# Products of ones at TensorE's waits in a threshold search, and twenty side products moved later

## The chip, the cores and the metric

The kernel runs on one core of one Trainium2 chip. The metric is the device time of one execution in microseconds. One core has five engines with queues of their own (TensorE, VectorE, ScalarE, GpSimd, SyncE) that meet at semaphores, and 16 DMA engines that are fed from queues of SyncE, ScalarE and GpSimd.

## The reference, cut to what is computed

```python
x = mlstm(q, k, v, i_gate, f_gate, o_gate)       # 3072 tokens x 320

# first mixture of experts: balanced, 8 experts, 384 tokens each
logits = x @ w_gate                               # 3072 x 8
order = np.argsort(-logits.flatten())
for idx in order:                                 # the greatest logit first
    tok, e = idx // E, idx % E
    if assigned[tok] >= 0 or counts[e] >= cap:
        continue
    assigned[tok] = e; counts[e] += 1
out[assigned == e] = relu(x[assigned == e] @ w1[e]) @ w2[e]

# second mixture of experts: x / |x| against expert_emb / |expert_emb|,
# argmax picks the expert, softmax gives its weight
out[idx == e] = gate_w * (relu(x[idx == e] @ w1[e]) @ w2[e])
```

## The kernel before, in words

It has four stages: the recurrence (mLSTM), the routing of the first mixture with its logits, the experts of the first mixture, the experts of the second. The change is in the routing alone.

The greedy assignment is done without a sort. It runs in 7 phases (`PHASES`). In a phase every token that is still free chooses its best open expert (VectorE, `keys`), and for each expert the smallest key that it can accept is searched 4 bits at a time in 8 rounds (`ROUNDS`). The 24 blocks of 128 tokens stand as 24 columns. One round is a ring between two engines:

- VectorE compares the keys with 16 candidates in three pieces, L1040, of 6, 10 and 8 blocks (`FIRST`, `cmp_ready`).
- TensorE counts: a product with the capacity, L1509, then 24 small products of 8 columns, L1513, each over one block of the comparison. The last one raises `cnt_ready`.
- VectorE tests the counts, L1074 (`kcol_ready`).
- TensorE turns the digits found into the next candidates: `digit`, L1497. Digits of earlier rounds of the same half (`q < r`) are added before the wait for `kcol_ready`, the new one behind it (`kb_ready`). In the first round of a half there is no earlier one, in its fourth there are three.
- VectorE compares against the result, which it reads from PSUM. In rounds 0 and 4 the candidates are a constant in SBUF instead.

After 8 rounds `settle` takes the tokens above the threshold and the ties in order. TensorE's part of it is `assign(0)` (L1475), a count (L1525), three products that rank the ties (L1528 to L1530) and one that sums them (L1531), then `assign(1)`.

Between these TensorE has side work, `side(count)`: 192 steps (L1489, two products of 8 columns each, which the trace shows as four records) that multiply the transposed `w2` of the first experts by the normalised embeddings of the second router. `made` counts them. Their operands come in 16 chunks of 12 steps, in four buffers. The last product of a chunk raises `w2t_used`, and SyncE loads chunk j into a buffer once `w2t_used` says that chunk j - 4 is done. After the last step ScalarE copies the sum (`w2e_ready`), which TensorE wants before it turns the rows of expert 0.

SyncE's queue is in order. Around the routing it holds: chunks 4, 5 and 6, the store of all tokens (`x_rows<-tokens`, L440), chunks 7 to 15, then the raw weights of expert 2 (L407 to L412). After the routing GpSimd gathers the rows of expert 0 (L731) by the order found, TensorE turns them (L1566) and the expert stage begins.

GpSimd splits the weights of experts 0 and 1 (L758 to L789) in two bursts during the routing.

`spin(dst, count)` (L1307 to L1310) issues products of a matrix of ones with 512 columns into a bank that nobody reads. Before the change it is used in the first 25 us alone. `bank[5]`, `bank[6]` and `bank[1]` are idle at the places where the change writes ones.

Of the kernel before, what the change touches and what calls it, by code (L numbers as in the profile page):

```python
# [87 lines left out]
def build(nc, t, out):  # L88
    ctx = ExitStack()
    with ctx:  # L90
# [196 lines left out]
        bank = [ctx.enter_context(nc.psum_tensor(f"bank{i}", [128, 512], fp32)) for i in range(8)]  # L287
# [1014 lines left out]
        def _(pe):  # L1302
# [4 lines left out]
            def spin(dst, count):  # L1307

                for _ in range(count):
                    T.matmul(dst[:, :], ones[:, :], ones[:, 0:1].to_broadcast([128, 512]), start=True, stop=True)  # L1310
# [158 lines left out]
            def ranks(src):  # L1469

                T.matmul(bank[4][:, 0:E * G], tri[:, :], src.rearrange("p e g -> p (e g)"), start=True, stop=False)
                return T.matmul(bank[4][:, 0:E * G], ones[:, :], prev_b.rearrange("p e g -> p (e g)"), start=False, stop=True)

            def assign(j, src, last=False):
                T.matmul(bank[0][:, 0:G * E], eye[:, j, :], src.rearrange("p g e -> p (g e)"), start=False, stop=last).then_inc(assigned_ready, 1)  # L1475
# [3 lines left out]
            def side(count):  # L1479

                if made[0] == 0:
                    pe.wait_ge(embT_done, 1)
                for m in range(made[0], made[0] + count):
                    f, k, j = m // KT, m % KT, m // (KT * FT // 2)
                    at = k * HF + f % (FT // 2) * 128
                    if m % (KT * FT // 2) == 0:
                        pe.wait_ge(ld_w2t[j % 4], 16 * (j // 4 + 1))
                    for rows in (slice(0, 64), slice(64, 128)):
                        last = T.matmul(bank[3][rows, f * E:(f + 1) * E], w2t[j % 4][:, at + rows.start:at + rows.stop], eg[:, k * E:(k + 1) * E],  # L1489
                                        start=(k == 0), stop=(k == KT - 1))  # L1490
                    if (m + 1) % (KT * FT // 2) == 0:
                        last.then_inc(w2t_used[j % 4], 1)
                made[0] += count

            def digit(q, last, r=None):
                r = q if last else r
                return T.matmul(threshold[r % 2][:, 0:WAYS], kcol[:, q:q + 1].to_broadcast([WAYS, 128]), kstep[:, last * ROUNDS + q, :],  # L1497
                                start=(q % (ROUNDS // 2) == 0), stop=bool(last))

            side(40)  # L1500
            pe.wait_ge(choice_ready, 1)
            T.matmul(bank[0][:, 0:G * E], eye[:, 0, :], over_b.rearrange("p g e -> p (g e)"), start=True, stop=False).then_inc(assigned_ready, 1)
            for ph in range(PHASES):
                for r in range(ROUNDS):
                    n = ph * ROUNDS + r
                    if r == 0:
                        pe.wait_ge(cap_ready, ph + 1)
                        pe.wait_ge(choice_ready, ph + 1)
                    T.matmul(bank[6][0:WAYS, 0:E], minus1[0:1, :], cap_eff[0:1, :], start=True, stop=False)  # L1509
                    for g in range(G):  # L1510
                        if g in FIRST:
                            pe.wait_ge(cmp_ready, PIECES * n + FIRST.index(g) + 1)
                        last = T.matmul(bank[6][0:WAYS, 0:E], cmp_b[:, g, :], choice[:, g, :], start=False, stop=(g == G - 1))  # L1513
                    last.then_inc(cnt_ready, 1)
                    for q in range(r // (ROUNDS // 2) * (ROUNDS // 2), r):
                        digit(q, 0, r)
                    pe.wait_ge(kcol_ready, n + 1)
                    digit(r, 1).then_inc(kb_ready, 1)
                    if r in (2, 5):
                        side(1)  # L1520
                side(3)
                pe.wait_ge(over_ready, ph + 1)
                assign(0, over_b)
                pe.wait_ge(osum_ready, ph + 1)
                T.matmul(bank[1][:, 0:E], ones[:, :], osum_b[:, :], start=True, stop=True).then_inc(over_count, 1)  # L1525
                side(2)
                pe.wait_ge(ties_ready, ph + 1)
                T.matmul(bank[4][:, 0:E * G], eye[:, 2, :], tie_b.rearrange("p e g -> p (e g)"), start=True, stop=False)  # L1528
                T.matmul(bank[4][:, 0:E * G], tri[:, :], tie_b.rearrange("p e g -> p (e g)"), start=False, stop=False)
                T.matmul(bank[4][:, 0:E * G], ones[:, :], prev_b.rearrange("p e g -> p (e g)"), start=False, stop=True)  # L1530
                T.matmul(bank[5][:, 0:E], ones[:, :], run_b[:, G - 1:E * G:G], start=True, stop=True).then_inc(rank_ready, 1)  # L1531
                side(3)
                pe.wait_ge(missed_ready, ph + 1)
                assign(1, missed_b)
                if ph < PHASES - 1:
                    side(7)
            pe.wait_ge(over_ready, PHASES + 1)
            assign(0, over_b, True)
            pe.wait_ge(ties_ready, PHASES + 1)
            ranks(chosen[:, :, :]).then_inc(rank_ready, 1)  # L1540
            side(20)
            for g in range(G):
                if g % (G // PIECES) == 0:
                    pe.wait_ge(lane_ready, g // (G // PIECES) + 1)
                last = T.matmul(bank[6][:, 0:2 * G], lane_is[:, g, :], place_of[:, g, :, :].rearrange("p a j -> p (a j)"), start=(g == 0), stop=(g == G - 1))
            last.then_inc(order_ready, 1)
# [215 lines left out]
```

## Time and profile before

| | before |
|---|---|
| times of 3 runs | 833.1, 836.4, 884.54 us; median 836.4 |
| the profiled execution | 834.51 us, its span 832.5 us |
| TensorE busy in the span | 732.9 us, 88% |
| mean granted TensorE clock | 0.875 |
| logits end, routing begins | 160.4 us |
| routing ends, rows of expert 0 turned | 320.2 us |

The profile is one execution. Its span runs from the first to the last instruction. Engines are called PE (TensorE), PEld (its weight loads), DVE (VectorE), ACT (ScalarE), POOL (GpSimd), SP (SyncE). A number in brackets behind a row is the time that the engine stood idle before it and what ended that. The granted clock is the share of 2.4 GHz that TensorE was given: 1.00 is 2.4 GHz, 0.50 is 1.2 GHz.

### The profile page before, as it was taken

What the parts mean: (1) busy time and instruction counts of PE and PEld (TensorE: products, weight loads), DVE (VectorE), ACT (ScalarE), POOL (GpSimd) and SP (SyncE); (2) the same over time, 40 slices, a digit from 0 to 9 for tenths busy, and PEclk for the clock granted to TensorE, in tenths of its full rate; (3) what the DMA queues carried; (4) which work ended last, traced back from release to release, by engine and by line L of the source; (5) the groups of instructions that cost most, each with busy time, mean ns of one, the idle gap of its engine ahead of it and who ended that gap; (6) DMA issues with size and microseconds to landing.
All of it is one profiled execution on the core that took longest, in us unless ns stands there. A gap on an engine that the chain in (4) does not pass through costs nothing.

```text
span 832.5 us, 21421 instructions
## 1 busy us (share of the span) xinstructions
PE 732.9 (88%) x7336; PEld 645.3 (78%) x7338; DVE 448.5 (54%) x1220; ACT 276.9 (33%) x625; POOL 419.0 (50%) x573
## 2 busy tenths in 40 slices
PE   7988889987888878999999999089999999999994
PEld 3677768975766757999999998068988988988994
DVE  7799997657666672366556665713222222222231
ACT  3444321000000002567666676323333332333330
POOL 4677772537000003578787766502644775347530
PEclk9999999855555556999999999689999999999997
DMA  5666685799321162335545533364749667642310
GB/s 170 205 220 206 224 272 155 187 311 331 101 80 67 41 178 58 99 99 191 168 128 186 188 122 107 113 176 122 231 131 299 189 209 224 189 133 80 111 56 0
DMA packets 66155, 132.28 MB, mean 159 GB/s; under 512 B 14743, under 2 KB 48432, under 8 KB 64306
## 3 DMA queue, kind: packets, MB, share of 16 engines
q1 hardware_dynamic: 45346, 84.85, 32.5%
q0 software_dynamic: 9600, 35.85, 13.9%
q10 hardware_dynamic: 11152, 10.82, 4.7%
q8 instruction: 36, 0.59, 0.3%
q14 instruction: 21, 0.17, 0.1%
HBM read 94.23 MB, written 15.34 MB: 132 GB/s over the span
## 4 chain that ended last, share of the span: by engine, by line
PE 60%; DVE 20%; issue 9%; ACT 3%; POOL 3%; DMA 2%; DVEq 1%; SPq 0%; ACTq 0%; POOLq 0%
PE bank L1552 10%; PE bank L1553 9%; PE bank L1554 9%; PE bank L1513 5%; PE bank L1579 3%; PE bank L1580 3%; PE bank L1581 3%; PE bank L1670 3%; DVE mlstm_arena L879 2%; PE bank L1445 2%; PE bank L1652 2%; PE bank L1651 2%; DVE routing_arena L1040 2%; PE bank L1489 2%; PE bank L1584 1%
## 5 line engine op out<-in xcount | busy, mean ns | idle before, releaser
L1552 PE MATMUL bank<-w_hi,hT_hi 128*128 (+1 forms) x440 | 141.2, 321 | 5.9 <-DVE hT_lo L1154 3.4
L1553 PE MATMUL bank<-w_lo,hT_hi 128*128 (+1 forms) x440 | 137.4, 312 | 0.0
L1554 PE MATMUL bank<-w_hi,hT_lo 128*128 (+1 forms) x440 | 137.1, 312 | 0.0
L789 POOL TENSOR_TENSOR w_lo<-w_raw,w_hi 128x320 fp32r<-128x320 f32 x128 | 109.0, 882 | 17.8 <-ACT w_hi L525 16.8
L758 POOL TENSOR_TENSOR w_lo<-w_raw,w_hi 128x256 fp32r<-128x256 f32 x128 | 94.8, 771 | 33.1 <-DMA w_hi<-w_raw 29.9
L1552 PEld LDWEIGHTS bank<-w_hi,hT_hi 128*128 128x128 f32 x440 | 83.3, 189 | 8.5 <-issue 8.4
L731 POOL DMA_INDIRECT routing_arena<-x_rows,routing_arena x24 | 23.3, 972 | 128.5 <-DVE routing_arena L1142 107.4
L1553 PEld LDWEIGHTS bank<-w_lo,hT_hi 128*128 128x128 f32 x440 | 83.4, 189 | 0.0
L1554 PEld LDWEIGHTS bank<-w_hi,hT_lo 128*128 128x128 f32 x440 | 83.3, 189 | 0.0
L1229 DVE TENSOR_TENSOR xT_lo<-bank,xT_hi 128x256 fp32r<-128x256 f32 x31 | 13.2, 425 | 113.4 <-ACT xT_hi L597 109.9
L1154 DVE SCALAR_TENSOR_TENSOR hT_lo<-bank,hT_hi 128x384 fp32r<-128x384 f32 x64 | 35.7, 558 | 69.5 <-ACT hT_hi L540 67.6
L593 ACT ACTIVATE routing_arena<-bank 128x512 f32<-128x512 f32 x62 | 36.8, 600 | 89.8 <-PE bank L1652 69.0
L611 ACT ACTIVATE hT_hi<-bank 128x512 fp32r<-128x512 f32 x62 | 33.7, 596 | 95.7 <-PE bank L1670 95.7
L1552 PE MATMUL bank<-w_hi,xT_hi 128*128 x124 | 52.0, 420 | 10.7 <-issue 6.7
L1241 DVE TENSOR_SCALAR tokens<-bank,routing_arena 128x320 f32 (+1 forms) x31 | 17.1, 551 | 82.2 <-PE bank L1554 77.7
L637 ACT ACTIVATE w_emb<-bank 128x512 f32<-128x512 f32 x1 | 0.6, 597 | 179.7 <-PE bank L1489 179.7
L879 DVE TENSOR_TENSOR_SCAN mlstm_arena<-bank,mlstm_arena 128x384 f32<-128x384 f32 x64 | 57.1, 935 | 2.4 <-PE bank L1326 2.4
L1513 PE MATMUL bank<-routing_arena 128*16 128x8 bf16 x1344 | 46.1, 167 | 10.9 <-DVE routing_arena L1040 10.3
L1513 PEld LDWEIGHTS bank<-routing_arena 128*16 128x16 bf16 x1344 | 39.1, 89 | 16.4 <-DVE routing_arena L1040 14.9
L834 POOL DMA_INDIRECT out<-tokens,routing_arena x31 | 30.7, 989 | 39.2 <-issue 23.1
L1554 PE MATMUL bank<-w_hi,xT_lo 128*128 x124 | 49.0, 395 | 0.0
L1553 PE MATMUL bank<-w_lo,xT_hi 128*128 x124 | 49.0, 395 | 0.0
(271 smaller groups left out, 1759.7 us busy)
## 6 DMA issues: line engine op xcount, KB each, us to landing
w_raw<-in_moe_w SPq DMA_DIRECT2D x16, 1280.0 KB, 6.8
w_raw<-in_moe_w SPq DMA_DIRECT2D x16, 1024.0 KB
w_hi<-w_raw POOLq DMA_DIRECT2D x8, 1280.0 KB, 6.8
turn_arena<-in_moe_w2t SPq DMA_DIRECT2D x12, 768.0 KB, 7.5
w_raw<-in_moe_w SPq DMA_DIRECT2D x32, 256.0 KB
w_hi<-w_raw POOLq DMA_DIRECT2D x8, 1024.0 KB, 8.2
routing_arena<-x_sorted ACTq DMA_DIRECT2D x31, 160.0 KB
w_hi<-w_raw POOLq DMA_DIRECT2D x16, 256.0 KB, 8.9
```

What stands on the lines that cost most here:

```text
L593: nc.scalar.activation(hid[:, f * 512:(f + 1) * 512], bank[f][:, :], ACT.Relu).then_inc(relu_done, 1)
L611: nc.scalar.activation(hT_hi[:, 4 * f:4 * f + 4, 0:128], bank[3 + f][:, :].rearrange("p (k t) -> p k t", k=4), ACT.Copy).then_inc(hh_ready, 1)
L758: last = nc.gpsimd.tensor_tensor(w1_lo[:, s, k, c], w1_raw[:, k, c], w1_hi[:, s, k, c], ALU.subtract)
L789: last = nc.gpsimd.tensor_tensor(w2_part(w2_lo, n)[:, k, :], w2_raw[:, k, :], w2_part(w2_hi, n)[:, k, :], ALU.subtract)
L834: pool.indirect_dma_start(out, bass.IndirectOffsetOnAxis(ap=ids[:, b:b + 1], axis=0), tokens[:, b, 0:DM], None, bounds_check=N - 1, oob_is ...
L879: V.tensor_tensor_scan(decay[:, h, c], bank[f][:, 0:HALF], diag[:, :], 0.0, ALU.mult, ALU.add).then_inc(decay_done, 1)
L1154: V.scalar_tensor_tensor(hT_lo[:, f, :], bank[f % 2][:, 0:BPE * 128], 0.0, hT_hi[:, f, :], ALU.max, ALU.subtract).then_inc(hl3_done, 1)
L1513: last = T.matmul(bank[6][0:WAYS, 0:E], cmp_b[:, g, :], choice[:, g, :], start=False, stop=(g == G - 1))
L1552: T.matmul(dst, a_hi, b_hi, start=first, stop=False)
L1553: T.matmul(dst, a_hi, b_lo, start=False, stop=False)
L1554: return T.matmul(dst, a_lo, b_hi, start=False, stop=last)
L1579: T.matmul(dst, w1_hi[:, s, k, cols], xT_hi[:, k, :], start=(k == 0), stop=False)
```

## The change

Products of ones (one product of 512 columns each) are put: between the side products at the front of the routing (five), before the wait for `kcol_ready` in every round, behind the new digit in the six rounds that have no side step there, and at three places of the settling part (two in the last phase). `side(40)` at the front becomes `side(20)` in portions of four. The other steps go: one more to each phase, four and four around the last assignment, two before each of two waits for `lane_ready`, one to the end.

```diff
-            side(40)
+            for _ in range(5):
+                side(4)
+                spin(bank[5], 1)
             pe.wait_ge(choice_ready, 1)
...
                     for q in range(r // (ROUNDS // 2) * (ROUNDS // 2), r):
                         digit(q, 0, r)
+                    spin(bank[5], 1)
                     pe.wait_ge(kcol_ready, n + 1)
                     digit(r, 1).then_inc(kb_ready, 1)
                     if r in (2, 5):
                         side(1)
+                    else:
+                        spin(bank[5], 1)
                 side(3)
                 pe.wait_ge(over_ready, ph + 1)
                 assign(0, over_b)
+                spin(bank[5], 1)
                 pe.wait_ge(osum_ready, ph + 1)
                 T.matmul(bank[1][:, 0:E], ones[:, :], osum_b[:, :], start=True, stop=True).then_inc(over_count, 1)
-                side(2)
+                side(3)
                 pe.wait_ge(ties_ready, ph + 1)
...
+                spin(bank[6], 1)
                 side(3)
                 pe.wait_ge(missed_ready, ph + 1)
                 assign(1, missed_b)
                 if ph < PHASES - 1:
-                    side(7)
+                    side(3)
+                    spin(bank[1], 1)
+                    side(4)
+                else:
+                    side(4)
             pe.wait_ge(over_ready, PHASES + 1)
             assign(0, over_b, True)
+            side(4)
             pe.wait_ge(ties_ready, PHASES + 1)
             ranks(chosen[:, :, :]).then_inc(rank_ready, 1)
             side(20)
             for g in range(G):
                 if g % (G // PIECES) == 0:
+                    if g:
+                        side(2)
                     pe.wait_ge(lane_ready, g // (G // PIECES) + 1)
```

## Rows read from the trace of the kernel before

**Rows 1.** The page: busy share in 40 slices of the span, and the granted clock

```profile
PE   7988889987888878999999999089999999999994
PEclk9999999855555556999999999689999999999997
```

**Rows 2.** Stretches: start:end, us, busy time of each engine, granted clock, DMA share, GB/s

```profile
155.00:160.00 5.00, 5.00 (x38) 4.40 (x35) 1.84 (x6) 0.00 (x0) 3.62 (x6) 1.00 0.63 137
160.40:169.00 8.60, 8.60 (x161) 8.58 (x160) 6.49 (x11) 0.00 (x0) 8.44 (x12) 0.50 0.29 89
170.44:182.40 11.96, 9.69 (x212) 7.98 (x214) 6.75 (x37) 0.00 (x0) 4.06 (x6) 0.50 0.91 295
16.84:20.25 3.41, 3.19 (x14) 1.83 (x15) 3.25 (x5) 0.00 (x0) 0.81 (x2) 0.50 0.25 77
```

**Rows 3.** Who waited for whom from 170 to 303 us: total us, times, longest

```profile
DVE routing_arena L1074 <- PE bank L1513: 28.6, 55, 3.1
DVE routing_arena L1040 <- PE bank L1497: 11.9, 42, 0.3
```

**Rows 4.** Timeline of two rounds: start us, us, engine, line, operation

```profile
170.44 0.19 PE L1497 MATMUL bank<-routing_arena 16*128 16x16 bf16 x1 [0.26 <-DVE routing_arena L1074]
170.67 0.68 DVE L1040 TENSOR_TENSOR routing_arena<-routing_arena,bank 128x96 bf16<-128x96 f32 x3 [0.28 <-PE bank L1497]
170.98 0.83 PE L1513 MATMUL bank<-routing_arena 128*16 128x8 bf16 x24 [0.20 <-DVE routing_arena L1040]
172.12 0.19 PE L1497 MATMUL bank<-routing_arena 16*128 16x16 bf16 x1 [0.19 <-DVE routing_arena L1074]
...
175.05 0.52 PE L1497 MATMUL bank<-routing_arena 16*128 16x16 bf16 x4
```

**Rows 5.** Timeline, TensorE in the first stage: ones at full and half clock

```profile
9.56 3.22 PE L1310 MATMUL bank<-ones 128*128 128x512 bf16 x14
...
19.04 3.19 PE L1310 MATMUL bank<-ones 128*128 128x512 bf16 x7 [0.22 <-POOL mlstm_arena L697]
```

**Rows 6.** Timeline of the settling part of phase 0

```profile
183.76 0.19 PE L1525 MATMUL bank<-routing_arena,ones 128*128 128x8 bf16 x1 [0.38 <-DVE routing_arena L1090]
...
184.53 0.34 PE L1528 MATMUL bank<-routing_arena 128*128 128x192 bf16 x1
...
185.24 0.16 DVE L1102 SCALAR_TENSOR_TENSOR routing_arena<-routing_arena,bank 128x8 f32<-128x8 f32 x1
...
187.91 0.70 DVE L1040 TENSOR_TENSOR routing_arena<-routing_arena 128x96 bf16<-128x96 f32 x3
188.23 0.84 PE L1513 MATMUL bank<-routing_arena 128*16 128x8 bf16 x24
```

**Rows 7.** Timeline of the front of the routing

```profile
160.37 2.73 PE L1489 MATMUL bank<-emb_weights,tokens 128*64 128x8 f32 x48
...
163.91 2.40 DVE L1040 TENSOR_TENSOR routing_arena<-routing_arena 128x96 bf16<-128x96 f32 x3
...
169.43 0.75 PE L1513 MATMUL bank<-routing_arena 128*16 128x8 bf16 x24
...
170.22 0.15 DVE L1074 TENSOR_SCALAR_CACHE_REDUCE routing_arena<-bank 16x8 f32<-16x8 f32 x1 [3.15 <-PE bank L1513]
```

**Rows 8.** Timeline of SyncE's DMA issues

```profile
174.06 24.11 SPq L440 DMA_DIRECT2D x_rows<-tokens  x2
...
296.20 1.54 SPq L407 DMA_DIRECT2D w_raw<-in_moe_w  x1
```

**Rows 9.** Stretches at the end of the routing, columns as in rows 2

```profile
304.50:310.00 5.50, 4.69 (x82) 4.40 (x82) 4.66 (x12) 0.00 (x0) 0.00 (x0) 0.50 1.03 253
314.45:320.19 5.74, 4.19 (x70) 3.92 (x68) 0.55 (x4) 0.60 (x1) 2.98 (x3) 0.50 0.38 106
```

**Rows 10.** Timeline of the end of the routing

```profile
303.63 0.34 PE L1475 MATMUL bank<-routing_arena 128*128 128x192 bf16 x1 [1.05 <-DVE routing_arena L1117]
...
320.19 2.18 PE L1566 MATMUL bank<-ident,routing_arena 128*128 128x128 f32 x9 [1.05 <-DMA routing_arena<-x_rows,routing_arena]
```

## The prediction

> **What bounds the kernel now.** I read the page first: its two lines of slices show the granted clock of TensorE at a half from slice 9 to slice 15, which is the routing, and at full before and after [rows 1]. Then the stretches, for what that clock goes with. TensorE is busy in all of 155 to 160 us at full clock, and in all of 160.4 to 169 us at half clock [rows 2], so the profile's busy share doesn't tell what holds the clock up. The difference is the work: the stretch at half clock is side products of 8 columns. Last the waits and the timeline. In the search VectorE waits 28.6 us for the counts and 11.9 us for the digits [rows 3]. Two rounds in order show the ring: digit at 170.44, compare at 170.67, 24 counts from 170.98, next digit at 172.12 [rows 4]. The 56 rounds and seven settling parts make up the time from 169.4 to about 303 us; everything that lengthens the ring moves the experts, where TensorE is nine tenths busy [rows 1], by as much. So the question is what 512 columns of ones cost in the ring, and whether they bring the clock back.
>
> **What a product of ones costs.** At full clock 14 of them took 3.22 us, at half clock 7 took 3.19 us [rows 5]. Without the drain of the last one (0.38 and 0.63 us, the modelled length of a single one) the spacing is 2.84 / 13 = 0.22 us and 2.56 / 6 = 0.43 us. TensorE's queue is in order: what stands behind the ones is the new digit in the first place, the 24 counts in the second, and VectorE waits for both.
>
> **Does the clock come back?** I take it that it does not. In a round there would be two products of ones, 0.86 us at half clock in a ring of some 2 us. The nearest row is 16.84 to 20.25 us: longer products, 3.19 us busy of 3.41, three of them ones, and the clock stays at 0.50 [rows 2], and further ones in a row follow [rows 5] before it rises. The denser stretch did not lift it, so I don't expect the sparser to. It is already low when the routing begins: it fell between 160.0 and 160.4 us, as logits products of 64 columns gave way to side products, without a gap on the engine [rows 2], and the change leaves the logits as they are.
> The Trainium skill, TensorE: Matmul & The Clock Gate, part 1, says that the slow clock is the default and that activity releases it; read as "stay busy" it speaks for this change and gives the first rival below. The trace doesn't agree with that reading: 8.60 us busy of 8.60 at a clock of 0.50 [rows 2].
>
> **The front.** A side step is four records, and 48 records took 2.73 us; less 0.25 for the drain that is 0.053 each, 0.21 us a step [rows 7]. Twenty steps and five ones are 4.2 + 2.1 = 6.3 us instead of 8.6. The first counts can start at 167.1 instead of 169.43. The compare before them ends at 163.91 + 2.40 = 166.31, so it doesn't hold them; VectorE's idle 3.15 us before 170.22 shows that it was free from 167.07 [rows 7]. Gain 2.3 us, at most 3.1.
>
> **Ones before the wait for the count.** The last of the 24 counts of the first round starts at 169.43 + 0.75 - 0.17 (its drain) = 170.01 [rows 7], and the digit follows 0.43 us behind it, at 170.44 [rows 4]. A product behind it starts about 0.10 us later, as the first old digit does. So the ones end 0.10 + 0.43 = 0.53 us behind the last count: 0.10 us late in the first round of a half. Each old digit ahead of them adds its spacing, (0.52 - 0.19) / 3 = 0.11 us [rows 4]: 0.21, 0.32 and 0.42 us in the other three. Sum 1.05 us a half, 2.1 a phase, 14.7 us in seven phases. The bounds are nothing (if the ones did slip under the wait) and 0.43 us in each round, 24 us.
>
> **Ones behind the digit.** The counts start 0.54 us after the digit (170.98 - 170.44) [rows 4]. Digit 0.11, ones 0.43 and the two records of the capacity product, some 0.06 us each as those of the side steps, make 0.66: 0.12 us late. After rounds 2 and 5 a side step stood there already and stays. After round 3 VectorE has to make the new key first and there is room. After round 7 it counts in the settling part. Four rounds a phase, 0.5 us, 3.4 us in all; bounds 0 and 56 x 0.12 = 6.7.
>
> **The settling part.** Ones and one more side step before the ranks are 0.43 + 0.21 = 0.64 us, of which 0.38 is idle time before L1525 now; the ranks start 0.26 us late. VectorE's L1102 at 185.24 begins as the sum L1531 arrives, with nothing to spare, so 0.26 us goes to VectorE [rows 6]. Two further ones, 0.86 us, stand before the counts of the next round at 188.23; TensorE has about 0.4 us of slack there, and the shift of VectorE gives another 0.26. Late by the counts: some 0.45 us. Six phases and 0.26 for the last, 3.0 us; bounds 0 and 7 x 1.3 = 9. The side steps around the last assignment and at the `lane_ready` waits are covered: TensorE is idle 1.05 us before 303.63 [rows 10] and as long behind it, and four steps are 0.85.
>
> **SyncE's queue.** The steps moved are also the ones that free its buffers. Chunk 11 is done after 144 steps. Before, the last phase begins with 40 + 6 x 17 = 142, and the raw weights of expert 2 are issued at 296.20 [rows 8]. Now it begins with 20 + 6 x 18 = 128, reaches 143 by its end, and the 144th stands behind the last assignment, now at 303.63 [rows 10]: the load is issued some 8 us later against the search. It and its chunk are 3.7 MB; at 253 GB/s, the rate at which the DMA engines are full at 304.5 to 310 [rows 9], that takes 14.5 us, until 318.6. The gather that TensorE waits for until 320.19 [rows 10] now has engines at 0.38 of their time [rows 9] and would share them. Its 0.6 MB behind the load would land at 320.9. I put 1 us, bounds 0 and 5. Chunk 6 and with it the store of the tokens leave at the end of phase 0 instead of 174.06 [rows 8]; nobody needs the store before the gather. It gives the DMA engines to GpSimd's weight copies, so GpSimd's second burst begins earlier. Its price on VectorE is a compare of 2.40 us [rows 7] instead of 0.70 [rows 6] when it meets round 0 or 4, wherever it lies: nothing, plus or minus 2 us.
>
> **Sum.** -2.3 + 14.7 + 3.4 + 3.0 + 1.0 = 19.8 us on the profiled 834.5 us: **854 us**. The profiled execution is 1.9 us below the median of the three runs, 836.4; a 2% change, about what a measurement of this kernel can tell from no change, ends at 851 from the one and 853 from the other.
>
> **The rivals.** *The clock is held at full through the search (not slower).* Then a digit or ones in the ring take 0.22 us, which fits both waits except in the fourth round of a half (0.06 us over, 14 times, 0.8 us). Counts gain little: the compare ends 0.68 us after its start, at 171.35 [rows 4], and eight counts follow it, so the last can start at best about 0.1 us before the 170.98 + 0.66 = 171.64 of now. 56 x 0.1 = 5.6 us. The front gains its 3.1. 834.5 - 5.6 + 0.8 - 3.1 + 1.0 = **828 us**. For it speaks that ones back to back did hold full clock in the first stage [rows 5]; against it the stretch at 16.84. *The clock is full in a part of the search* and falls in the settling parts: about the middle, **841 us**. Between full and half, the time is no longer than before once some three rounds in four run at full clock. *The load hits the gather fully*: the rows land last, 5 us late instead of 1, **858 us**; the DMA engines' full share of 1.03 before speaks for it, that descriptors of two queues can alternate against it.
>
> **How the numbers follow.** Half clock with the sum as it stands 0.66, with the gather late 0.08, clock full 0.13, in part 0.13. The predicted time is the first. The first alone has 846 to 862, since its three ring terms share one bound-to-bound uncertainty. The range of 829 to 862 takes in the partial case and the upper half of the full one. Slower by over 2%: seven tenths of the half-clock cases, 0.52. Faster by over 2% would need 817 to 820, beyond even the full-clock sum: 0.03. Within 2%: 0.45.
>
> **What would show it.** Granted clock still 0.50 from 165 to 320 us; the product of ones 0.63 us long; L1497 behind the wait later by 0.1 to 0.4 us and the round near 2.0 us instead of 1.68 (172.12 - 170.44) [rows 4]; first L1074 at about 168; L407 of expert 2 after the last assignment; DMA share near 1 while the gather runs. A granted clock of 1.00 between 170 and 300 us would make the prediction wrong at its second step, and rounds under 1.68 us would follow.

## The result, and the profile after

| | before | after |
|---|---|---|
| times of 4 runs | 833.1, 835.9, 836.4, 884.5 us | 863.8, 863.9, 871.1, 889.7 us |
| median | 836.2 | 867.5 |
| profiled execution, its span | 834.51, 832.5 | 871.07, 869.1 |
| TensorE busy in the span | 732.9, 88% | 792.7, 91% |
| mean granted TensorE clock | 0.875 | 0.857 |

The change makes the kernel slower: ratio after to before 1.037, 95% interval 1.029 to 1.046. One run of each kernel, 884.5 and 889.7 us, belongs to a slower kind and is not in the ratio. The forecast was 854 us with a range of 829 to 862, so the direction was right and the time lies above the range.

Line numbers from 1502 on have moved: the counts are L1515, the capacity product L1511, the new ones L1310, the count in the settling part L1531, the sum of the ranks L1537, the turned rows L1580; the first product behind the front, which waits for `choice_ready`, was L1502 and is L1504. L1497, L1475, L1489, L1040 and L1074 are as before.

The page of after, busy share and granted clock in 40 slices:

```profile
PE   7898889998999999899999999629999999999994
PEclk8799999855555555599999999959999999999998
```

TensorE is now at nine tenths or more in nearly every slice of the routing, and its clock is at 5 there as it was [rows 1]. Filling the waits did not bring the clock back.

Stretches of after (columns as in rows 2 of before): the front, the first rounds, a later phase, the gather:

```profile
167.24:176.00 8.76, 8.76 (x114) 6.10 (x113) 5.83 (x13) 0.00 (x0) 8.60 (x12) 0.50 0.23 67
176.00:190.00 14.00, 14.00 (x206) 8.21 (x206) 6.72 (x35) 0.00 (x0) 6.10 (x9) 0.50 0.91 300
311.00:335.00 24.00, 24.00 (x348) 15.36 (x349) 12.65 (x64) 0.00 (x0) 0.00 (x0) 0.50 0.10 34
345.00:356.00 11.00, 9.80 (x174) 9.24 (x172) 7.22 (x17) 0.00 (x0) 2.83 (x3) 0.50 1.00 325
```

In the second and third TensorE shows no idle time at all, where in the first rounds it had been busy for 9.69 us of 11.96 [rows 2]. The ring has changed its bound: it was the trip between two engines, and is now TensorE's queue.

The waits of after, 177 to 320 us (as rows 3 of before; us in total, times, longest):

```profile
DVE routing_arena L1074 <- PE bank L1515: 28.6, 46, 1.1
DVE routing_arena L1040 <- PE bank L1497: 20.7, 35, 0.6
```

VectorE's wait for a digit was at most 0.3 us [rows 3] and is now up to 0.6.

The timeline of TensorE in after, the front and the first rounds (start us, us, engine, line, operation):

```profile
167.24 1.03 PE L1489 MATMUL bank<-emb_weights,tokens 128*64 128x8 f32 x16
168.19 0.61 PE L1310 MATMUL bank<-ones 128*128 128x512 bf16 x1
...
174.19 0.61 PE L1310 MATMUL bank<-ones 128*128 128x512 bf16 x1
174.59 0.37 PE L1504 MATMUL bank<-routing_arena 128*128 128x192 bf16 x1
...
175.73 0.61 PE L1310 MATMUL bank<-ones 128*128 128x512 bf16 x1
176.27 0.19 PE L1497 MATMUL bank<-routing_arena 16*128 16x16 bf16 x1
176.39 0.61 PE L1310 MATMUL bank<-ones 128*128 128x512 bf16 x1
176.93 0.22 PE L1511 MATMUL bank<-routing_arena 1*16 1x8 f32 x2
...
179.91 0.22 PE L1497 MATMUL bank<-routing_arena 16*128 16x16 bf16 x2
180.06 0.61 PE L1310 MATMUL bank<-ones 128*128 128x512 bf16 x1
```

Take differences of starts. From a product of ones to the digit behind it: 176.27 - 175.73 = 0.54 us. From ones to the capacity product: 176.93 - 176.39 = 0.54. From ones to L1504: 174.59 - 174.19 = 0.40. The forecast had 0.43 for all of them. Two old digits in a row reach the ones behind them 0.15 us after the first of them (180.06 - 179.91).

The weight loads (PEld) of two products that stand behind ones, and the count L1531 in a settling part, whose weights are the ones again but in a load of its own:

```profile
174.21 0.12 PEld L1504 LDWEIGHTS bank<-routing_arena 128*128 128x128 bf16 x1
176.26 0.10 PEld L1497 LDWEIGHTS bank<-routing_arena 16*128 16x128 bf16 x1 [0.44 <-DVE routing_arena L1074]
...
267.26 0.63 PE L1310 MATMUL bank<-ones 128*128 128x512 bf16 x1
267.31 0.11 PEld L1531 LDWEIGHTS bank<-routing_arena,ones 128*128 128x128 bf16 x1
267.69 0.21 PE L1531 MATMUL bank<-routing_arena,ones 128*128 128x8 bf16 x1
```

Where the load starts while the ones run (174.21, 267.31), the product follows them at 0.40 or 0.43 us. Where it starts only as they are through (176.26), the product follows at 0.54.

One whole phase of after on VectorE: its first three tests and its last, then the first of the next phase:

```profile
250.46 0.15 DVE L1074 TENSOR_SCALAR_CACHE_REDUCE routing_arena<-bank 16x8 f32<-16x8 f32 x1 [1.08 <-PE bank L1515]
252.49 0.15 DVE L1074 TENSOR_SCALAR_CACHE_REDUCE routing_arena<-bank 16x8 f32<-16x8 f32 x1 [0.58 <-PE bank L1515]
254.64 0.15 DVE L1074 TENSOR_SCALAR_CACHE_REDUCE routing_arena<-bank 16x8 f32<-16x8 f32 x1 [0.69 <-PE bank L1515]
...
265.11 0.15 DVE L1074 TENSOR_SCALAR_CACHE_REDUCE routing_arena<-bank 16x8 f32<-16x8 f32 x1 [0.69 <-PE bank L1515]
...
273.83 0.15 DVE L1074 TENSOR_SCALAR_CACHE_REDUCE routing_arena<-bank 16x8 f32<-16x8 f32 x1 [1.08 <-PE bank L1515]
```

The first two rounds take 2.03 and 2.15 us, all seven intervals of the phase 14.65, and the way to the next phase 8.72. The same view of before, in its first phase:

```profile
173.53 0.15 DVE L1074 TENSOR_SCALAR_CACHE_REDUCE routing_arena<-bank 16x8 f32<-16x8 f32 x1 [0.49 <-PE bank L1513]
175.16 0.15 DVE L1074 TENSOR_SCALAR_CACHE_REDUCE routing_arena<-bank 16x8 f32<-16x8 f32 x1 [0.49 <-PE bank L1513]
...
181.96 0.15 DVE L1074 TENSOR_SCALAR_CACHE_REDUCE routing_arena<-bank 16x8 f32<-16x8 f32 x1 [0.49 <-PE bank L1513]
189.10 0.15 DVE L1074 TENSOR_SCALAR_CACHE_REDUCE routing_arena<-bank 16x8 f32<-16x8 f32 x1 [0.40 <-PE bank L1513]
```

There a round takes 1.63, the phase 181.96 - 170.22 [rows 7] = 11.74 (11.68 in the later ones), and the way to the next 7.14.

Two views of one line give the length of the search in every kernel of this study: the tests, L1074, and the order at the end, L1142 (times, shortest, median and longest in ns, first and last start in us). After:

```profile
L1074 DVE TENSOR_SCALAR_CACHE_REDUCE routing_arena<-bank x56: 147/154/155, 175.8 to 335.2; 16x8 f32<-16x8 f32 x56
L1142 DVE SCALAR_TENSOR_TENSOR routing_arena<-bank,turn_arena x1: 183/183/183, 352.1 to 352.1; 128x24 int32<-128x24 f32 x1
```

Before:

```profile
L1074 DVE TENSOR_SCALAR_CACHE_REDUCE routing_arena<-bank x56: 147/154/155, 170.2 to 298.3; 16x8 f32<-16x8 f32 x56
L1142 DVE SCALAR_TENSOR_TENSOR routing_arena<-bank,turn_arena x1: 182/182/182, 314.0 to 314.0; 128x24 int32<-128x24 f32 x1
```

From the first test to the order: 352.1 - 175.8 = 176.3 us against 314.0 - 170.2 = 143.8, 32.5 us more. This number, called the search below, is the measure of the experiments, since it leaves out the first stage, whose clock is not the same in all executions although none of its instructions was changed: between 30 and 60 us it was 1.00 in the trace of before and 0.83 in that of after. There the first side product came at 167.24 instead of 160.37 [rows 7], 6.9 us later, before any instruction that was changed.

So the 36.6 us between the two spans are: first stage +6.9, front -1.25 (first side product to first test 8.60 instead of 9.85), search +32.5, order to the turned rows +0.1 (358.4 - 352.1 against 320.19 - 314.0), experts -1.6. The search itself: 7 x 2.97 = 20.8 in the rounds, 6 x 1.57 + 1.2 = 10.6 between the last test of a phase and what follows, and the 1.1 left is GpSimd's second burst, which lies elsewhere. While the burst runs, VectorE's operations take longer (in before L1086 takes 1.15 us at 203.18 and 0.56 at 261.44), so its price depends on which of them it meets: beyond the usual lengths of a phase and of the way to the next it is 3.4 us in before and 4.5 in after.

### The profile page after: what moved, and what is told of

It reads as the page before. It is cut to its first block, busy times and chain, and to the rows that moved or that the text cites. A ratio compares the mean times of both kernels' runs of the same rounds, so it can differ in the third digit from the quotient of the medians.

```text
span 869.1 us, 21668 instructions
## 1 busy us (share of the span) xinstructions
PE 792.7 (91%) x7460; PEld 660.8 (76%) x7461; DVE 449.6 (52%) x1220; ACT 276.7 (32%) x625; POOL 418.7 (48%) x573
## 4 chain that ended last, share of the span: by engine, by line
PE 69%; DVE 12%; issue 7%; DMA 3%; ACT 3%; POOL 3%; DVEq 1%; ACTq 0%; SPq 0%; POOLq 0%
PE bank L1566 9%; PE bank L1567 9%; PE bank L1568 9%; PE bank L1310 7%; PE bank L1515 4%; PE bank L1489 4%; PE bank L1593 3%; PE bank L1594 3%; PE bank L1595 3%; PE bank L1684 3%; PE bank L1445 2%; DVE mlstm_arena L879 2%; PE bank L1666 2%; PE bank L1665 2%; PE bank L1497 2%
## 5 line engine op out<-in xcount | busy, mean ns | idle before, releaser
L1310 PE MATMUL bank<-ones 128*128 128x512 bf16 x173 | 90.5, 571 | 1.5 <-POOL ones L650 1.5
L1593 PE MATMUL bank<-xT_hi,w_hi 128*128 128x384 f32 x128 | 45.3, 354 | 1.2 <-issue 1.2
```

The source lines that it names most:

```text
L1593: T.matmul(dst, w1_hi[:, s, k, cols], xT_hi[:, k, :], start=(k == 0), stop=False)
```

## The experiments

Each experiment is a kernel of its own; all but the first were run once. The kernel before varies by more than 10 us from run to run, so their whole times say little about a few us, and the search, the rounds and the way to the next phase are what is compared. The first five experiments tell the places apart, the next three are about the clock, the last two about the size of a product.

**Only the moved steps, no ones.** `side(20)` at the front and the other moved steps as in the change, none of the ones.

```diff
-            side(40)
+            side(20)
...
-                side(2)
+                side(3)
```

> The side products moved as in the change, no product of ones added. Theory 1 (the ones cost the time, the moves nothing or a little): the front gains 2.5 to 3 us, the ranks of seven settling parts start up to 0.2 us later each (1.4 us), GpSimd's second burst comes earlier (about 1 us): 831 to 835 us, within 0.5% of before. Theory 2 (the moves and SyncE's queue cost a part of the 30 us): 840 us or more, seen as a longer settling part or as a later gather.

Measured in ten runs: median 832.5 us against 840.2 for the kernel before on the same chip; ratio 0.993, interval 0.988 to 0.998. Its search goes from 175.1 to 321.3: 146.2 us, 2.4 more than before, of which 1.8 is GpSimd's burst, that now lies over more of a settling part (6.6 us behind the last test of its phase instead of 4.8), and 0.6 the extra step in the settling part (7.24 instead of 7.15 us a phase). The front gives 3.4 (first side product at 168.65, first test at 175.14); what the first test waits for there is VectorE's compare, which ends at 174.47. So the trace shows a gain of 1.0 us. The ratio stands for some 5.7, which the trace doesn't explain; the lowest times of the two kernels, 830.9 and 833.5, are 2.5 apart. The moved steps are a small gain at most, and no part of the loss beyond the 2.4.

**Only the ones, no steps moved,** in the rounds and the settling parts:

```diff
+                    spin(bank[5], 1)
                     pe.wait_ge(kcol_ready, n + 1)
                     digit(r, 1).then_inc(kb_ready, 1)
...
+                    else:
+                        spin(bank[5], 1)
...
                 assign(0, over_b)
+                spin(bank[5], 1)
...
+                spin(bank[6], 1)
...
+                    spin(bank[1], 1)
```

> Before, with the products of ones in the rounds and the settling part, and no side product moved (none of the ones at the front). Theory 1: the eight tests of a phase span 14.65 us as in the changed kernel instead of 11.68, the settling parts are 1.4 us longer: 860 to 866 us. Theory 2: 850 us or less.

Measured: 860.8 us; rounds of a phase 14.65 us, as in after; first test 169.2, order 341.1, a search of 171.9, +28.1. The way to the next phase is 8.51 us, 1.36 more than before; GpSimd's burst costs 1.4 less.

**Only the ones before the wait for the count.**

```diff
+                    spin(bank[5], 1)
                     pe.wait_ge(kcol_ready, n + 1)
```

> Ones only ahead of the wait for the count. Theory 1 (the instruction behind a product of ones starts 0.53 us after it, not 0.43): digits 0.20, 0.33, 0.35 and 0.38 us later in the four rounds of a half, 2.5 us a phase, 17.7 us in all: 851 to 854 us. Rival (only the 0.43 us of streaming count, as predicted): 0.10 to 0.42 us, 14.7 us: 849 us. Rival (it fits under the wait): 835 us.

Measured: 852.1 us. VectorE's timeline in it, the first four tests of one phase:

```profile
238.90 0.15 DVE L1074 TENSOR_SCALAR_CACHE_REDUCE routing_arena<-bank 16x8 f32<-16x8 f32 x1 [0.40 <-PE bank L1513]
240.74 0.15 DVE L1074 TENSOR_SCALAR_CACHE_REDUCE routing_arena<-bank 16x8 f32<-16x8 f32 x1 [0.39 <-PE bank L1513]
242.70 0.15 DVE L1074 TENSOR_SCALAR_CACHE_REDUCE routing_arena<-bank 16x8 f32<-16x8 f32 x1 [0.49 <-PE bank L1513]
244.68 0.15 DVE L1074 TENSOR_SCALAR_CACHE_REDUCE routing_arena<-bank 16x8 f32<-16x8 f32 x1 [0.50 <-PE bank L1513]
```

From test to test it takes 1.84, 1.96, 1.98, and 2.31 us (fourth to fifth, 1.92 before): 0.21, 0.33, 0.36 and 0.39 us late. A phase of rounds is 13.88 us (+2.20), the way to the next 7.53 (+0.38, the lateness of the eighth round), the search 161.8 (171.3 to 333.1), +18.0.

**Only the ones behind the digit.**

```diff
                     if r in (2, 5):
                         side(1)
+                    else:
+                        spin(bank[5], 1)
```

> Ones only behind the new digit. Theory 1: the counts start 0.26 us later, run without waiting for the compare and are 0.18 us late in rounds 1, 2, 5 and 7, 0.7 us a phase: 5 us, 839 to 841 us. Rival (as predicted, 0.12 us in four rounds): 838 us. Rival (hidden behind the compare): 835 us.

Measured: 838.2 us; four intervals of a phase 1.82 instead of 1.63, the others unchanged, 12.46 us a phase (+0.78) and 7.15 to the next. 7 x 0.78 = 5.5; the search is 148.2, +4.4, since GpSimd's burst cost 1.0 less here. So 838 us, the time of the rival with 0.12 us, is luck: the lateness is that of the first theory. 2.20 + 0.78 = 2.98: the two places add up to the 2.97 of after, with nothing between them.

**Only the ones in the settling part.**

```diff
                 assign(0, over_b)
+                spin(bank[5], 1)
...
+                spin(bank[6], 1)
                 side(3)
...
-                    side(7)
+                    side(3)
+                    spin(bank[1], 1)
+                    side(4)
```

> The products of ones in the settling part alone (three a phase, two in the last), nothing in the rounds or at the front, no step moved. Theory (each product holds what stands behind it by some 0.54 us of TensorE's half clock, and only the slack that was there is free): the rounds stay at 11.68 us; from the last L1074 of a phase to the first of the next 7.15 becomes 8.0 to 8.2, since of the 8.51 measured with ones at all places some 0.38 came with the ones before the wait in the rounds (7.53 without the others); first side product to end 672.2 becomes some 678 to 679. Rival, the settling part has slack for them as the prediction had it (0.45 a phase, of which a part from the rounds): 7.15 becomes at most 7.4 and the sum 674.

Measured: 840.5 us; rounds 11.68, the way to the next phase 7.82, the search 147.9 (174.8 to 322.7), +4.1. That is 0.67 a phase: more than the forecast's 0.45, less than the 0.85 to 1.05 that I then expected. Neither of the two expectations was right. Added up, the 1.57 us of the settling part of after are 0.38 from the rounds, 0.67 from its own ones, 0.09 from the step, and 0.43 that no single part shows. Where it arises is shown by the kernel with all the ones and no step moved, 8.51: 0.31 come as the ones of the rounds and those of the settling part meet (8.51 - 7.15 - 0.38 - 0.67), and 0.12 more as the step joins them (8.72 - 8.51 = 0.21 instead of 0.09). The likely reason is slack that each of them fits into alone and that they use up together; which wait it is was not tried.

**A burst of ones ahead of the front,** added to the kernel after. Is a denser stretch at the start what the clock lacks?

```diff
+            spin(bank[5], 16)
             for _ in range(5):
                 side(4)
```

> The changed kernel with a burst of 16 products of ones in a row ahead of its front, so that the search begins at full clock. Theory 1 (the ones in the rounds are too sparse to hold the clock): granted clock 1.00 behind the burst, back at 0.50 within the first phases, the later phases at 14.65 us between the first and the last test; 3 to 6 us more than the changed kernel, 866 to 876 us. Rival (they hold it once it is up): 1.00 until about 300 us, phases of 11.5 us or less, 835 us or less.

Measured: 864.2 us, a little under the 866 to 876 expected. Stretches:

```profile
163.10:168.00 4.90, 4.65 (x98) 3.57 (x99) 3.42 (x5) 0.00 (x0) 4.82 (x7) 1.00 0.41 130
170.00:330.00 160.00, 141.64 (x2140) 98.04 (x2171) 87.51 (x417) 0.00 (x0) 19.47 (x26) 0.50 0.35 108
```

The clock stays at 2.4 GHz over the front and falls to 1.2 as the rounds begin (first test at 168.53), ones and all. The rounds take 14.65 us a phase as in after, 14.55 in the first. So it isn't only that the clock was low when the routing began.

**Three products of ones at both places of the rounds,** from the kernel after:

```diff
-                    spin(bank[5], 1)
+                    spin(bank[5], 3)
                     pe.wait_ge(kcol_ready, n + 1)
...
-                        spin(bank[5], 1)
+                        spin(bank[5], 3)
```

> The changed kernel with three products of ones instead of one at each place in the rounds. Theory 1 (half clock throughout): 14 places a phase, two more at 0.43 us each, 12 us a phase: 84 us more, some 948 us. Rival (denser ones lift the clock): granted clock 1.00 in the search, three products at 0.22 us delay a digit by about 0.3 us and the counts by about 0.25: phases of 15 to 16 us, 870 us. This shows what the clock wants and what a round costs at full clock, not a version to keep.

Measured: 944.6 us, near the 948 of half clock, but not for its reason. Stretches:

```profile
205.00:220.00 15.00, 14.34 (x140) 6.32 (x140) 3.65 (x21) 0.00 (x0) 2.92 (x5) 0.50 1.06 291
300.00:320.00 20.00, 18.78 (x297) 11.47 (x302) 8.83 (x51) 0.00 (x0) 0.00 (x0) 1.00 0.20 67
```

With so many ones the clock is full in stretches: the first two phases run at 0.50 with 24.79 us of rounds, the fourth at 1.00 with 16.94, the others between. Even at full clock the phase is 5.3 us longer than with no ones at all, since three of them still take 0.75 us ahead of what waits behind (304.48 - 303.73):

```profile
303.73 0.82 PE L1310 MATMUL bank<-ones 128*128 128x512 bf16 x3
304.48 0.20 PE L1511 MATMUL bank<-routing_arena 1*16 1x8 f32 x2
```

**What would full clock be worth?** The kernel with the moved steps alone, and 16 ones right ahead of the first count:

```diff
             side(20)
+            spin(bank[5], 16)
             pe.wait_ge(choice_ready, 1)
```

> The side products moved, none of the ones in the rounds, but a burst of 16 ones right before the first count. Theory 1: the burst costs 3.5 to 7 us at the front; the first rounds run at full clock and are no more than 0.15 us shorter than 1.63 us each, then the clock falls: 836 to 840 us. Rival (the ring is bound by TensorE's clock): the rounds at full clock are 0.3 us or more shorter.

Measured: 860.1 us instead of the 836 to 840 expected; the granted clock was 0.50 from 60 to 90 us, and the first side product came at 182.2 us. The stretch of the burst's end and the first round, and the one behind:

```profile
192.00:195.80 3.80, 3.17 (x60) 2.14 (x59) 1.12 (x8) 0.00 (x0) 2.75 (x5) 0.95 0.55 102
196.00:210.00 14.00, 11.75 (x227) 9.72 (x228) 9.01 (x45) 0.00 (x0) 2.46 (x4) 0.50 1.25 328
```

TensorE in it (columns as above):

```profile
193.06 0.75 PE L1514 MATMUL bank<-routing_arena 128*16 128x8 bf16 x24
...
194.06 0.18 PE L1497 MATMUL bank<-routing_arena 16*128 16x16 bf16 x1 [0.26 <-DVE routing_arena L1074]
...
194.59 0.83 PE L1514 MATMUL bank<-routing_arena 128*16 128x8 bf16 x24 [0.21 <-DVE routing_arena L1040]
...
195.68 0.19 PE L1497 MATMUL bank<-routing_arena 16*128 16x16 bf16 x1
```

The round begun at 194.06, nearly all of it at full clock, takes 1.62 us; the rounds at half clock take 1.63. The 24 counts show 0.83 us here as at half clock [rows 4], and where they wait for nothing, at 193.06, 0.75 us as at half clock too [rows 7]. So the small bf16 products of the ring last no longer at 1.2 GHz. (The fp32 side products do: 16 records take 0.64 us at full clock, in the kernel with the burst at the front, and 1.03 at half; but they are not in the ring's path.) In the rounds as they are before the change, full clock brings no time, or a hundredth of a us: the aim of the change had nothing behind it there. That rests on one round at full clock. Of a settling part without ones at full clock no run has a row. Where ones stand, full clock does take back a part of their own price: in the kernel with three of them the way to the next phase is 7.63 us in a stretch at 1.00 (350.3 to 358.0) against 8.72 in after, still more than the 7.15 of before.

**Ones of 64 columns** at both places of the rounds, in the kernel before:

```diff
+                T.matmul(dst[:, 0:64], ones[:, :], ones[:, 0:1].to_broadcast([128, 64]), start=True, stop=True)
```

> Before, with products of ones of 64 columns instead of 512 at both places of the rounds, nothing moved. Theory 1 (the price is the streaming plus 0.1 us to the next weight load, less the slack of the wait): 0.05 + 0.11 us fits under both waits, at most 0.03 us in the third and fourth round of a half: 834 to 836 us, phases of 11.7 to 11.8 us. Rival (any product there costs a fixed 0.2 us): phases of 13 us or more, 845 us.

Measured: 861.1 us, from which nothing can be read directly, since the clock was 0.50 from 60 to 118 us and the first side product came at 190.5. The search is 145.2 (198.7 to 343.9), +1.4, of which GpSimd's burst is 1.1; a phase of rounds 11.72. The clock is 0.50 in all of it.

**Ones of 256 columns** before the wait alone, to try the size of the term:

```diff
+                T.matmul(dst[:, 0:256], ones[:, :], ones[:, 0:1].to_broadcast([128, 256]), start=True, stop=True)
```

> Products of ones of 256 columns instead of 512 before the wait for the count in every round, nothing else. At 1.2 GHz 256 columns take 0.21 us instead of 0.43. Theory (a fixed part of about 0.11 us for the weight load behind the ones stands on top of the columns, and the ring waits for what ends behind the last count): lateness 0.21 us less than with 512 columns in every round, so a first round of a half nearly unchanged at 1.63 and the others some 0.12 to 0.17 late; a phase 12.3 to 12.5 us of rounds instead of 13.88 (512 columns) and 11.68 (none); the sum about 5 us over the kernel before. Rival, the lateness goes with the columns alone: half of the 2.20 us a phase, 12.8 us. Second rival, the ring loses a fixed amount for any product put there: near 13.5 us. Under every one of them the granted clock stays at 0.50 in the search.

Measured: 840.8 us. The first four tests of a phase:

```profile
250.61 0.15 DVE L1074 TENSOR_SCALAR_CACHE_REDUCE routing_arena<-bank 16x8 f32<-16x8 f32 x1 [0.40 <-PE bank L1518]
252.23 0.15 DVE L1074 TENSOR_SCALAR_CACHE_REDUCE routing_arena<-bank 16x8 f32<-16x8 f32 x1 [0.39 <-PE bank L1518]
253.98 0.15 DVE L1074 TENSOR_SCALAR_CACHE_REDUCE routing_arena<-bank 16x8 f32<-16x8 f32 x1 [0.49 <-PE bank L1518]
255.75 0.15 DVE L1074 TENSOR_SCALAR_CACHE_REDUCE routing_arena<-bank 16x8 f32<-16x8 f32 x1 [0.50 <-PE bank L1518]
```

And TensorE in one round:

```profile
202.50 0.39 PE L1315 MATMUL bank<-ones 128*128 128x256 bf16 x1
202.83 0.19 PE L1502 MATMUL bank<-routing_arena 16*128 16x16 bf16 x1
```

Rounds of 1.62, 1.75 and 1.77 us: the first is not late, the next two are by 0.12 and 0.14; 12.39 us a phase (+0.71), as the fixed part on top of the columns says, and not the 12.8 of columns alone. The search is 150.4 (167.9 to 318.3), +6.6. The ones hold the digit for 0.33 us (202.83 - 202.50), 0.21 less than with 512 columns: 256 columns at 1.2 GHz take 0.21 (half of the 0.43 of 512), so some 0.12 of either time does not go with the columns.

## Why the prediction was right and wrong

**Right: the clock does not come back.** It is 0.50 throughout the search, with TensorE busy in 24.00 us of 24.00 from 311 to 335. The rival of 828 us was mis-argued too: its gain of 5.6 us at full clock is nothing by the round at 194.06.

**Right in mechanism, mis-sized: "Ones before the wait for the count".** 14.7 us on record, 18.0 measured, by the kernel with these alone. The lateness in the four rounds was put at 0.10, 0.21, 0.32 and 0.42 us and measured 0.21, 0.33, 0.36 and 0.39. There are two errors. A product of ones was given its spacing among its like, 0.43 us, but what stood behind it was something else, whose weight load had not started under the ones: 0.54. And each old digit was given 0.11 us from a record of four that took 0.52 [rows 4]; that record held three old ones and the new one behind the wait, and so a part of the wait. The first old digit costs 0.12 (0.33 - 0.21), each further one only 0.03. The errors partly cancel.

**"Ones behind the digit".** 3.4 us on record, 5.5 measured (four intervals of 0.19 instead of 0.12). The four rounds named were the right ones. The error is again the 0.54 for 0.43, with 0.03 more for the digit and the capacity product (177.07 - 176.93 = 0.14 for the latter), less what the counts make up: they run without a gap in 0.75 us instead of 0.83.

**The step that failed most: "The settling part".** 3.0 us on record, 7.9 measured: 6 x (1.57 - 0.39) + (1.2 - 0.4). In after VectorE's L1102 waits for the sum where it had waited for nothing. One row shows it:

```profile
194.67 0.16 DVE L1102 SCALAR_TENSOR_TENSOR routing_arena<-routing_arena,bank 128x8 f32<-128x8 f32 x1 [0.51 <-PE bank L1537]
```

0.5 us instead of the 0.26 forecast, and the first test of the next phase waits 1.08 us for its counts instead of 0.40, 0.68 more where 0.19 was forecast (250.46 above). I had each product of ones at 0.43 where two of the three cost 0.51 and 0.54 (269.62 - 269.11 and 271.93 - 271.39), and credited 0.4 us of slack before those counts that the ones and the late sum together use up. The stacking, 0.43 us a phase that neither the ones nor the steps nor the rounds show by themselves, is the part that a sum over single edits can't see.

**"The front".** -2.3 on record, -1.25 measured. The first counts could start once 20 steps and five ones were through: 7.35 us (174.59 - 167.24) instead of 6.3. Per group of four steps 0.95 us (168.19 - 167.24) instead of 0.84, and 0.54 for the ones instead of 0.43, as in the rounds. With the ones left out, the front gives 3.4.

**"SyncE's queue".** The load of expert 2 is issued after the last assignment, as forecast, and the DMA share is 1.00 from 345 to 356 us, in which the gather begins. The row:

```profile
342.80 0.43 SPq L407 DMA_DIRECT2D w_raw<-in_moe_w  x1
```

Yet the turned rows come 6.3 us after the order instead of 6.2: +0.1 where 1.0 was forecast. The gather begins at 352.56, nearly 10 us behind that issue. From 345 to 350 us alone the DMA engines moved 374 GB/s, 1.9 MB of the load's 3.7, so by an estimate most of it had gone by. GpSimd's burst cost 1.1, inside the 0 plus or minus 2, though by more than the compare that the prediction named: it slows the settling part as well.

**The sum.** -1.25 + 18.0 + 5.5 + 7.9 + 0.1 + 1.1 = 31.4 us on 834.5 is 866, and with the experts' 1.6 us less 864.3. The shortest times measured are 863.8 and 863.9; the profiled one, 871.1, had 6.9 us more in its first stage. The forecast sum was 19.8. Of the 11.6 between, 4.9 is the settling part, 5.4 the two ring terms, 1.3 the rest. The range failed for a reason of its own. The prediction says that the three ring terms share one uncertainty, and gives them upper bounds of 24, 6.7 and 9 us, 18.6 above what the sum takes for them; yet its upper end, 862, leaves 8. One number, 0.43, stood in all three, so their errors had the same sign.

## What to carry to other kernels

Cost filler by the start of what stands behind it in the same queue, not by the spacing of filler among itself; here that was 0.54 us against 0.43, and it came back in every term, so such a number widens the range of the sum and not only of its term. Filler at several places of one queue can cost more than the places one by one, as in the settling part. Before buying clock, look at what it buys: if the operations of the path last the same at both clocks, as these small bf16 products do, a higher clock has no value there. What this change had to give lies in the moves alone (20 side steps taken out of the front: 1.0 us by the trace, ratio 0.993 by ten runs).

## What the runs showed of the hardware

- The granted clock was 0.50 with TensorE busy in 24.00 us of 24.00 (311 to 335 us of after, with 512 columns of ones between groups of 24 products of 8). It was 0.50 as well from 170 to 330 us of the kernel with the burst at the front; with up to six products of ones a round instead of two it was 0.50 from 205 to 220 us and 1.00 from 300 to 320.
- At 1.2 GHz a product of 512 columns holds the next one for 0.54 us where that one's weight load starts only behind it, and 0.32 at 2.4 (163.97 - 163.65 in the kernel with the burst at the front), where its like follow at 0.43 and 0.22; behind 256 columns it is 0.33. Where the records show the next weight load starting under the ones it is 0.40 (L1504) and 0.43 (L1531). So the 0.1 us on top of the columns goes with a weight load that is not done ahead; no run changed that alone.
- 24 bf16 products of 8 columns that wait for nothing took 0.75 us at either clock (193.06 in the kernel with the burst before the first count, 169.43 [rows 7]); 16 records of fp32 products took 0.64 us at full clock and 1.03 at half.
- A burst of 16 ones ahead of small products is followed by a few us at full clock, and then 0.50 again (1.00 from 163.10 to 168.00, 0.50 from 170 in one kernel; 0.95 from 192.00 to 195.80, 0.50 from 196 in another).
- The clock of the first stage is not the same in all executions, though its instructions are: between 60 and 90 us it was 1.00 in the traces of before and after, and 0.50 in the one with 64-column ones, whose first side product came at 190.5 us instead of 160.4.
